# Complex-rotation mixing stage of an fp32 transformer block: written out by batch, with token products between the theta products

## What is computed

```
theta = x @ w_theta
y[b] = w_tok_r @ (x * cos(theta))[b] + w_tok_i @ (x * sin(theta))[b]
u = x + y
out = u + max(u @ w_ch, 0)
```

## Time and profile before

| | |
|---|---|
| device time, median of 3 runs | 830.54 us (829.87 to 830.96) |
| span of the profiled execution, first to last instruction | 834.7 us |
| mean granted TensorE clock over the span | 0.920 |
| TensorE busy | 712.2 us (85%) |
| VectorE, ScalarE, GpSimd busy | 391.7, 296.8, 285.9 us |
| mixing stage in the span | from 597.3 to 834.7 us |

### The profile page before, as it was taken

One profiled execution on the slowest core, in us unless ns is written; L12 is line 12 of the kernel. 1 busy time (PEld: TensorE's weight loads), 2 busy tenths in 40 slices (PEclk: granted clock), 3 DMA queues, 4 the chain that ended last, 5 costly groups with the idle time before them and its releaser, 6 DMA issues. The chain is left out here.

```text
span 834.7 us, 11494 instructions
## 1 busy us (share of the span) xinstructions
PE 712.2 (85%) x3946; PEld 618.6 (74%) x3947; DVE 391.7 (47%) x573; ACT 296.8 (36%) x420; POOL 285.9 (34%) x212
## 2 busy tenths in 40 slices
PE   2899999999999989407999999999564679999997
PEld 1799999999999979405777777777453457888885
DVE  7666566665666401512343443433268996111111
ACT  2334443344433413203445354543235754111100
POOL 2123232232322215353354544533175755111100
PEclk9999999999999965557999999999877899999998
DMA  5034533354333107333655556441161001111000
GB/s 133 1 98 149 142 99 97 97 153 139 97 97 97 61 23 281 101 151 97 232 178 200 187 189 215 164 151 39 51 196 69 0 1 36 65 64 64 25 25 25
DMA packets 50075, 89.52 MB, mean 107 GB/s; under 512 B 17280, under 2 KB 17280, under 8 KB 50048
## 3 DMA queue, kind: packets, MB, share of 16 engines
q1 hardware_dynamic: 48128, 82.87, 31.2%
q0 software_dynamic: 1920, 6.29, 2.3%
HBM read 63.98 MB, written 25.17 MB: 107 GB/s over the span
## 5 line engine op out<-in xcount | busy, mean ns | idle before, releaser
L361 PEld LDWEIGHTS pv<-v_ones,probs 128*128 128x128 f32 x1152 | 146.7, 198 | 1.2 <-ACT probs L232 1.2
L361 PE MATMUL pv<-v_ones,probs 128*128 128x65 f32 x1152 | 144.0, 277 | 0.9 <-ACT probs L232 0.9
L839 POOL TENSOR_TENSOR w_lo<-stage,w_hi 128x1024 fp32r<-128x1024 f32 x28 | 90.0, 3217 | 107.3 <-ACT w_hi L834 107.1
L321 DVE TENSOR_REDUCE row_max<-ring 128x1 f32<-128x768 f32 x96 | 86.5, 951 | 9.7 <-PE ring L391 8.7
L232 ACT ACTIVATE probs<-ring 128x768 f32<-128x768 f32 x96 | 71.2, 812 | 23.3 <-PE ring L424 22.0
L879 DVE TENSOR_TENSOR ht_lo<-ht_ps,ht_hi 128x512 fp32r<-128x512 f32 x32 | 22.1, 691 | 106.2 <-ACT ht_hi L868 106.2
L157 POOL TENSOR_TENSOR k_lh<-k_raw,k_aug 64x768 fp32r<-64x768 f32 x16 | 32.8, 2052 | 105.2 <-DVE k_aug L272 105.2
L391 PE MATMUL ring<-k_aug,q_aug 96*128 96x384 f32 x192 | 57.6, 386 | 8.0 <-DVE row_max L321 6.8
L934 PE MATMUL down<-w_hi,ht_hi 128*128 128x512 f32 x128 | 52.9, 413 | 9.0 <-DVE ht_lo L879 9.0
L834 ACT CAST w_hi<-stage 128x1024 fp32r<-128x1024 f32 x56 | 58.7, 1048 | 0.0
L1144 ACT CAST m_xt_hi<-m_tp 128x512 fp32r<-128x512 f32 x24 | 13.9, 579 | 123.7 <-PE m_tp L1306 123.7
(11 more groups left out here) (190 smaller groups left out, 1381.2 us busy)
## 6 DMA issues: line engine op xcount, KB each, us to landing
stage<-in_w SPq DMA_DIRECT2D x64, 512.0 KB, 6.4
x_slots<-zeros SPq DMA_DIRECT2D x7, 1024.0 KB, 5.4
y_slots<-zeros SPq DMA_DIRECT2D x7, 1024.0 KB, 5.2
q_raw<-in_qT SPq DMA_DIRECT2D x32, 192.0 KB, 5.3
k_raw<-in_kT SPq DMA_DIRECT2D x32, 192.0 KB, 4.6
x_all<-x_slots SPq DMA_DIRECT2D x18, 256.0 KB, 2.7
wt_raw<-in_w_tok SPq DMA_DIRECT2D x6, 768.0 KB, 4.3
y_slots<-x_all SPq DMA_DIRECT2D x16, 256.0 KB, 6.8
```

What stands on the lines that cost most here:

```text
L321: nc.vector.tensor_reduce(row_max[:, j:j + 1], ring[j % 3][:, :, 0:HALF], AX.XY, ALU.max).then_inc(s_max, 1)
L361: last = nc.tensor.matmul(pv[:, t * (D + 1):(t + 1) * (D + 1)], probs[:, k, t * P:(t + 1) * P], v_ones[p][:, k, :], start=k == 0, stop=k = ...
L839: name.tensor_tensor(w_lo[w][:, r, :], stage[:, r, :], w_hi[w][:, r, :].bitcast(F32), ALU.subtract).then_inc(done, 1)
```

## The change

The two sections are joined, and all loops are written out. The token products are ordered by batch: n = 0 to 5 are the output tiles of batch 0, n = 6 to 11 those of batch 1. While the thetas are made, TensorE adds each finished tile s of batch 0 to the outputs 0 and 1 (`from_tile`), and from the ninth theta on it makes a whole output (`tokens`) after each theta. There are four PSUM banks for `y`, and `ch` uses the banks of `theta`.

The columns of the token matrices are loaded, cast and subtracted for every n: 12 times each, into three buffers instead of two. The first subtraction is on VectorE, the rest are on GpSimd. The gated tile, `u` and the result all lie in `x_tok`; the copies `x_now` and `x_mul` are gone. `turns` lies in `z[0]`, so ScalarE's `turn(c)` waits until both `z_lo` of tile c-2 are done. GpSimd makes the last four gathers after the products of the first tiles.

The diff, cut to its core:

```diff
@@ -985,27 +985,24 @@
-    x_now = [sb(f"x_now{q}", [P, DM]) for q in range(2)]
-    x_mul = [sb(f"x_mul{q}", [P, DM]) for q in range(2)]
-    turns = sb("turns", [P, DM])
...
-    wt_hi = [sb(f"wt_hi{q}", [P, 2, T, P], F32R) for q in range(2)]
-    wt_lo = [sb(f"wt_lo{q}", [P, 2, T, P], F32R) for q in range(2)]
+    wt_hi = [sb(f"wt_hi{q}", [P, 2, T, P], F32R) for q in range(3)]
+    wt_lo = [sb(f"wt_lo{q}", [P, 2, T, P], F32R) for q in range(3)]
...
-    y = [ps(f"y{b}", [P, DM]) for b in range(2)]
-    ch = [ps(f"ch{b}", [P, DM]) for b in range(2)]
+    y = [ps(f"y{q}", [P, DM]) for q in range(4)]
+    ch = theta
...
     def _(sp):
+        def load_wt(i):
+            if i > 0:
+                sp.wait_ge(s_wth, i)
+                sp.wait_ge(s_wtl, i)
+            sp.dma_start(wt_raw[:], w_tok[i % T, :, :, :, :]).then_inc(s_wt, 16)
...
+        for i in range(1, NC):
+            load_wt(i)
         rows = out.rearrange("b (t p) d -> b t p d", p=P)
+        for n in range(NC):
+            sp.wait_ge(s_o, n + 1)
+            sp.dma_start(rows[n // T, n % T, :, :], x_tok[:, n, :]).then_inc(s_out, 16)
...
     def _(pool):
+        for c in range(8):
+            gather(c)
+        for c in range(NC):
...
+            times_x(c)
+            if c + 8 < NC:
+                gather(c + 8)
+            if c in (0, 3):
+                columns_low(1 + c // 3)
+            if c in (7, 9, 10, 11):
+                columns_low({7: 3, 9: 4, 10: 5, 11: 6}[c])
+        for i in range(7, NC):
+            columns_low(i)
...
     def _(act):
+        def turn(c):
+            q = c % 2
+            act.wait_ge(s_th, c + 1)
...
+            if c >= 2:
+                act.wait_ge(s_zl, 2 * c - 2)
+            nc.scalar.activation(z[0][q][:], theta[q][:], ACT.Identity, bias=rounder[:],
+                                 scale=0.15915494309189535).then_inc(s_turn, 1)
...
+        for c in range(NC):
+            if c + 1 < NC:
+                x_high(c + 1)
+            if c >= 2:
+                z_high(c - 2)
+            turn(c)
+            if c >= 1:
+                waves(c - 1)
+            if c in (1, 3):
+                columns_high(c // 2 + 1)
+            if c >= 8:
+                columns_high(c - 5)
+        z_high(NC - 2)
+        waves(NC - 1)
+        z_high(NC - 1)
...
         high(wm_hi[:], w_raw[:], s_whi)
+        columns_high(7)
+        columns_high(8)
+        for n in range(NC):
+            x_high(NC + n)
+            if n in (1, 3, 5):
+                columns_high(9 + n // 2)
...
     def _(dve):
+        for c in range(NC):
+            if c + 1 < NC:
+                x_low(c + 1)
+            if c == 8:
+                add_x(0)
+                add_x(1)
+            if c >= 9:
+                add_x(c - 7)
+            if c + 3 < NC:
+                gated(c + 3)
+            if c >= 2:
+                z_low(c - 2)
+            reduce_angle(c)
...
     def _(pe):
+        def tokens(n):
+            pe.wait_ge(s_wtl, n + 1)
+            if n >= 4:
+                pe.wait_ge(s_u, n - 3)
+            for s in range(T):
+                from_tile(n, s)
...
+        for s in range(T):
+            turn_x(s + 3)
+            angles(s + 2)
+            if s == 0:
+                pe.wait_ge(s_wtl, 1)
+            from_tile(0, s)
+            if s == 0:
+                pe.wait_ge(s_wtl, 2)
+            from_tile(1, s)
+        turn_x(9)
+        angles(8)
+        tokens(2)
+        turn_x(10)
+        angles(9)
+        tokens(3)
+        turn_x(11)
+        angles(10)
+        tokens(4)
+        angles(11)
+        tokens(5)
+        tokens(6)
+        turn_u(0)
+        turn_u(1)
+        tokens(7)
+        for n in range(NC):
+            channels(n)
+            if n + 2 < NC:
+                turn_u(n + 2)
+            if n % 2 == 1 and n < 8:
+                tokens(8 + n // 2)
```

More of the change, by code:

```diff
@@ L1031, in mixing @@
     s_u = sem("m_u")
-    s_ut = sem("m_ut")
-    s_uh = sem("m_uh")
-    s_ul = sem("m_ul")
     s_ch = sem("m_ch")
     s_o = sem("m_o")
[L1037 to L1041, removed]
+    s_out = sem("m_out")
     block = ctx.enter_context(nc.Block())
[L1044 to L1075, removed]
     @block.sync
     def _(sp):
[L1079 to L1084, removed]
+        def load_wt(i):
[3 more added lines that the diff above has]
+            sp.dma_start(wt_raw[:], w_tok[i % T, :, :, :, :]).then_inc(s_wt, 16)
         load_wt(0)
@@ L1169, in waves @@
             nc.scalar.activation(z[0][q][:], z[0][q][:], ACT.Sin, bias=half_pi[:], scale=-1.0).then_inc(s_sin, 1)
[L1171 to L1196, removed]
+        act.wait_ge(s_wraw, 16)
+        high(wm_hi[:], w_raw[:], s_whi)
+        x_high(0)
+        columns_high(0)
+        for c in range(NC):
[13 more added lines that the diff above has]
+        z_high(NC - 1)
+        act.wait_ge(s_wraw, 32)
         act.wait_ge(s_th, NC)
-        act.wait_ge(s_wraw, 32)
         high(wm_hi[:], w_raw[:], s_whi)
[L1201 to L1209, removed]
+        columns_high(7)
[4 more added lines that the diff above has]
+                columns_high(9 + n // 2)
     @block.vector
@@ L1221, in gated, with x_low, z_low, reduce_angle @@
             nc.vector.tensor_scalar(x_tok[:, c, :], x_tok[:, c, :], gate[:, c:c + 1], None, ALU.mult).then_inc(s_gated, 1)
[L1223 to L1240, removed]
+        def x_low(k):
+            dve.wait_ge(s_xh, k + 1)
+            low(xt_lo[k % 2][:], tp[k % 2][:], xt_hi[k % 2][:], s_xl)
+        def z_low(c):
             for at, m in enumerate((1, 0)):
                 dve.wait_ge(s_zh, 2 * c + at + 1)
[L1243 to L1253, removed]
+                low(z_lo[:, c, m, :], z[m][c % 2][:], z_hi[:, c, m, :], s_zl)
+        def reduce_angle(c):
+            q = c % 2
+            turns = z[0][q]
             dve.wait_ge(s_turn, c + 1)
@@ L1267, in step @@
             nc.vector.tensor_scalar(angle[q][:], angle[q][:], BELOW_PI, -BELOW_PI, ALU.min, ALU.max).then_inc(s_r, 1)
[L1268 to L1279, removed]
-            dve.wait_ge(s_y, 2 * t + b + 1)
-            nc.vector.tensor_tensor(u[b][:], x_tile(b * T + t), y[b][:], ALU.add).then_inc(s_u, 1)
@@ L1341, in mix @@
-        def mix(t, q, b):
-            n = 2 * t + b
-            first = is_first(n)
-            pe.wait_ge(s_wtl, t + 1)
-            products = [(m, s, k) for s in range(T) for m in range(2) for k in range(3)]
-            for at, (m, s, k) in enumerate(products):
-                if at == len(products) // 3 and not first:
-                    channels(n - 1, 1 - b, 0)
-                if is_first(t) and m == 0 and k == 0:
-                    pe.wait_ge(s_zl, 2 * (b * T + s + 1))
-                a, w = PARTS[k]
-                last = nc.tensor.matmul(y[b][:], (wt_hi, wt_lo)[a][q][:, m, s, :],
-                                        (z_hi, z_lo)[w][:, b * T + s, m, :],
-                                        start=at == 0, stop=at == len(products) - 1)
-            last.then_inc(s_y, 1)
-            if not first:
-                channels(n - 1, 1 - b, 1)
@@ L1360, in _, with transpose, turn_x, project @@
[L1360 to L1362 removed]
+        def transpose(src, k):
+            for d in range(KD):
+                last = nc.tensor.transpose(tp[k % 2][:, d * P:(d + 1) * P], src[:, d * P:(d + 1) * P], ident[:])
+            last.then_inc(s_tp, 1)
+        def turn_x(c):
+            pe.wait_ge(s_gated, c + 1)
+            transpose(x_tok[:, c, :], c)
+        def project(dst, k, done):
+            pe.wait_ge(s_xl, k + 1)
+            for d in range(KD):
+                for n, (a, w) in enumerate(PARTS):
+                    last = nc.tensor.matmul(dst[:], (xt_hi, xt_lo)[a][k % 2][:, d * P:(d + 1) * P],
+                                            (wm_hi, wm_lo)[w][:, d, :], start=d == 0 and n == 0,
+                                            stop=d == KD - 1 and n == 2)
+            last.then_inc(done, 1)
@@ new lines, in angles, with from_tile @@
+        def angles(c):
+            if c == 0:
+                pe.wait_ge(s_wlo, 1)
+            if c >= 2:
+                pe.wait_ge(s_r, 4 * c - 6)
+            project(theta[c % 2], c, s_th)
+        def from_tile(n, s):
+            c = n // T * T + s
+            for m in (1, 0):
+                if n % T in (0, 1):
+                    pe.wait_ge(s_zl, 2 * c + 2 - m)
+                for k, (a, w) in enumerate(PARTS):
+                    last = nc.tensor.matmul(y[n % 4][:], (wt_hi, wt_lo)[a][n % 3][:, m, s, :],
+                                            (z_hi, z_lo)[w][:, c, m, :], start=s == 0 and m == 1 and k == 0,
+                                            stop=s == T - 1 and m == 0 and k == 2)
+            if s == T - 1:
+                last.then_inc(s_y, 1)
```

169 lines of the change are left out of this document (75 added, 94 removed).

## The result

| | before | changed |
|---|---|---|
| device time, median of 19 runs each | 830.54 us | 834.43 us |
| ratio, with its 95% interval | | 1.0048 (1.0032 to 1.0063) |
| span of the profiled execution | 834.7 us | 837.7 us |
| mixing stage, from ScalarE's first cast to the end of the span | 233.8 us | 236.9 us |

The change made the kernel 0.5% slower. Forecast were 827.2 us and 0.57 for faster. So stages are compared from that cast on.

The account below looks back on a forecast made before the run. Bound by VectorE and its waits for GpSimd in the theta section, by TensorE's work in the token section. 673.9 + 128.9 + 21.0 + 4.4 + 3.2 = 831.4 us of span, 3.3 less, so 827.2 us; range 819 to 836.

Parts of the forecast that it names:

- `turn(3)` starts: Mixing stage, ScalarE's turn of tile 3: forecast at 637 in span time, 36.1 us from the first cast.
- `turn(3)` to `turn(7)`, with one subtraction of columns: Theta section: four periods of 7.1 us, 28.4, plus GpSimd's column subtraction, about 3.0, and ScalarE's cast, 0.2.
- `turn(7)` to the end of theta 8: Theta section, TensorE: theta of tile 8 ends 5.3 us later, at 673.9, after 24 products and transposes.
- stalls before the outputs 4, 5, 6: TensorE after theta 8 waits for columns GpSimd subtracts behind tiles' products: 8.6, 8.0 and 4.4 us, together 21.0.
- half clock behind them: TensorE behind the three stalls: 1.7, 1.7 and 1.0 us lost, together 4.4; bounds for each 0 and 2.8.
- output 7 waits for columns: TensorE before output 7: no wait forecast, columns there at A+75.7, TensorE at A+76.4, A being theta 8's end.
- The start: Stage start to 637: nothing on the path changes up to GpSimd's first pair; later gather, columns and 8.1 us on TensorE.
- half clock behind output 6's stall: TensorE behind the third stall, 4.4 us long: 1.0 us lost to half clock.
- The period: Theta section, one `turn` to the next: 7.1 us against 6.66 before; second `angle` and clamp wait for GpSimd.
- The first rival: Theta section, VectorE not held by GpSimd: period 6.0 us, time 820.8 us; chance 0.15.
- Half clock: Rival, theta section: TensorE's clock falls and sets the period; 8.9 us gives 834, all half clock 847; chance 0.22.
- Slower: Whole kernel: measured slower than before, chance 0.26, of which the rival of half clock in the theta section has 0.22.

Follow-up runs that it names:

- a5_wch_later: Changed kernel with the 1 MB load of `w_ch` moved behind the sixth load of token columns: 830.66 us, 0.9987 of the kernel before.
- b1_loads_early: Kernel before, without SyncE's wait for the twelve gathers ahead of the loads of the first token columns and `w_ch`: 829.28 us, 0.9983.
- a3_cols_early: Changed kernel with GpSimd's subtractions of columns 4, 5 and 6 behind the products of tiles 8, 9, 10 instead of 9, 10, 11: 811.12 us, 0.9756.
- a4_turns_own: a5_wch_later with `turns` of tiles 0 to 9 in the unused `w_raw`, so `turn(c)` does not wait for `z_lo` of tile c-2: 834.34 us, 1.0046.
- d1_first_stall_only: Changed kernel with only GpSimd's subtraction of columns 4 moved, from behind the products of tile 9 to behind those of tile 8: 820.07 us, 0.9863.
- c2: c1 with the subtractions of columns 1 and 2 on VectorE instead of GpSimd: 802.54 us, 0.9655 of the kernel before.
- c1: Changed kernel with the edits of a3_cols_early and a5_wch_later together: 808.03 us, 0.9714 of the kernel before.
- c3: c2 with the edit of a4_turns_own as well: 805.48 us, 0.9695 of the kernel before.

## Why the prediction was wrong

The sum was 831.4 us of span against 834.7, or a stage of 230.5 us from ScalarE's first cast; 236.9 were measured. The direction hung on 3.3 us, and the sum was 6.4 off. By its own steps, each from the first cast:

| step | predicted | measured |
|---|---|---|
| `turn(3)` starts | 36.1 | 40.1 |
| `turn(3)` to `turn(7)`, with one subtraction of columns | 31.6 | 31.9 |
| `turn(7)` to the end of theta 8 | 5.3 | 5.6 |
| stalls before the outputs 4, 5, 6 | 8.6, 8.0, 4.4 | 8.4, 7.9, 4.3 |
| half clock behind them | 1.7, 1.7, 1.0 | 1.7, 1.7, 3.1 |
| output 7 waits for columns | no | no |

- **The start** is the step that failed. "Up to GpSimd's first pair nothing on the path changes" was said with GpSimd, ScalarE and VectorE in mind. SyncE's queue had lost its wait for the gathers, and I called the loads free on the ground of the late outputs alone. The bytes of `w_ch` went beside the second gather, which landed 2.9 us later. With only that load moved away, `turn(3)` came at 36.8, and the time was that of the kernel before. What followed on TensorE was not as told either. The sum starts it at 28.1 from the first cast, when the columns for output 1 are subtracted, with six products left; in fact no token product ran before 31.1 (27.9 in a5_wch_later), as TensorE waited for `z_lo` of tile 0, which VectorE could do only after a gate multiplication held up by that subtraction (3.92 us). Then all 12 products ran at half clock, 5.3 us up to the transposes, and theta at full clock, 2.8 instead of 4.2. By luck these errors nearly cancel: to `turn(3)` it was 9.1 us where the sum has 8.1.
- **The half clock behind output 6's stall** is a term of the right kind with the wrong size, 1.0 against 3.1. The bounds were 0 and 2.8, from the 12 products of the tail; here the first 13 products ran at half clock, up to 749.9. The stall was the shortest of the three, and I charged it least; it was the dearest. No run shows a rule for this term: the same stalls were followed by other stretches of half clock in other runs, and the tail itself ran at full clock in b1_loads_early. With the start put right the sum would still have been 2.9 us too low (230.5 against a5_wch_later's 233.4), most of it this term, and the forecast of a gain would still have failed.
- **The period** was right with its reason: 6.9 to 7.4 us against 7.1 (10.5 against 10.3 with the columns), `turns` free, the second `angle` and the clamp held. The Trainium skill's rule on shared interfaces (GPSIMD Engine Reference, section 8) told which operations would wait, and the rows agree: 0.69 for the first `angle`, which reads PSUM, 1.29 for the second.
- **The stalls** were right to 0.2 us each, and they and their half clock cost 27.1 us, of which a3_cols_early got 22.5 back. Here went the expected gain: TensorE had done 72 token products when theta 8 was ready, 16.3 us of work, and then stood for 20.6 us.
- **The rivals.** Half clock did not set the period in the theta section; the clock was 0.95 there. It came once between `turn(3)` and `turn(7)`, behind TensorE's wait of 4.3 us in the tile of the columns. "Slower" had a chance of 0.26 for other reasons than the one that held. The first rival's period of 6.0 came in some tiles of a4_turns_own, by another edit, and the kernel was slower.

## What to carry to other kernels

When a wait is taken out of a DMA queue, ask what moves up with it: a load that no one needs for 100 us still takes its share of the DMA engines from the gather that everyone needs (here 2.9 us for 1 MB). In a queue that works in order, place each step by the time at which its inputs are ready, not beside the step it resembles; three subtractions, each moved by one place, were worth 22 us. When two versions are compared, look at TensorE's clock behind each wait first: here it moved single products' stretches by 1.4 to 2.8 us between kernels that did the same work there. And an engine whose instruction holds up another's to its end (0.48 us became 3.9 to 4.1 here) is best given the long ones only when the other is idle.

## What was not expected of the hardware

- A wait that looks like a bubble can pay. The wait of `turn` for `z_lo` costs VectorE 0.82 us a tile, and both times that it was removed the theta section became longer (by 2.9 us to the start of output 2, and by 2.1).
- The idle time alone doesn't give the price of a wait of TensorE in half clock. A stall of 4.25 us was followed by 5.8 us at half clock, two of about 8 us by some 3.3 us each, and the second of these in d1_first_stall_only by 5.7. Output 7's wait of 2.1 us cost nothing in c2 and 1.6 to 1.7 us in a3, c1 and c3. The last channel product ran at 5.50 us in the kernel before and at 3.03 in b1_loads_early, behind the same work and waits. What decides it no run here shows.
- VectorE's subtraction of 128x1536 took 1.75 us and GpSimd's 3.43 to 4.2, and for that long a multiplication of 0.48 us on VectorE was held.
- The device time was 1.7 to 1.8 us above the span in every profiled execution whose time is listed (837.7 and 839.53 us in the changed kernel). By that the profiled execution of the kernel before took about 836.5 us and was one of its longer ones, and the 4.2 us by which the prediction put its median below the span are not a constant. The forecast went by a difference of spans, so this doesn't touch it.
